# Attention's value products placed behind the next tile's scores and ahead of the transposes

## The reference

```python
scores = scale * np.matmul(q, k.transpose(0, 1, 3, 2)) + bias     # per head, 576 x 576
attn = np.exp(scores - max); attn = attn / (attn.sum(-1, keepdims=True) + 1e-9)
x = np.matmul(attn, v)                                            # B, S, H*D = 4, 576, 512
logits = x @ w_gate; gate = sigmoid(x @ w_local)
# per batch, token by token: the expert is argmax(logits), or the previous token's where gate >= 0.5
out[b, s] = p[e] * (relu(x[b, s] @ w1[e]) @ w2[e])
```

## Time and profile before

| what | value |
|---|---|
| median of 3 runs | 714.79 us (714.54 to 715.71) |
| the profiled execution | 715.85 us, of which the span of instructions is 714.1 us |
| PE busy | 658.3 us (92% of the span) |
| DVE, ACT, POOL busy | 376.8, 343.8, 194.1 us |
| copy_a on DVE (L813) | 686 ns each |
| copy_shared on ACT (L630) | 266 ns each |

### The profile page before, as it was taken

One profiled execution on the slowest core, in us unless ns is written; L12 is line 12 of the kernel. 1 busy time (PEld: TensorE's weight loads), 2 busy tenths in 40 slices (PEclk: granted clock), 3 DMA queues, 4 the chain that ended last, 5 costly groups with the idle time before them and its releaser, 6 DMA issues. The chain is left out here.

```text
span 714.1 us, 14144 instructions
## 1 busy us (share of the span) xinstructions
PE 658.3 (92%) x4353; PEld 528.3 (74%) x4353; DVE 376.8 (53%) x803; ACT 343.8 (48%) x727; POOL 194.1 (27%) x178
## 2 busy tenths in 40 slices
PE   6777899999999999999955899999999999999994
PEld 3224788888888888888735788888888888888883
DVE  5999565555555555556657642478424422122220
ACT  4997566666666666666530341466424422212221
POOL 4000614444444444445501011112111111111101
PEclk9999999999999999999975899999999999999998
DMA  7778534447444444444074941148310011111100
GB/s 166 202 195 206 109 68 100 99 97 212 98 100 96 99 97 98 98 101 94 18 264 151 344 152 64 45 154 308 104 44 31 35 44 44 44 44 44 44 0 1
DMA packets 67960, 77.05 MB, mean 108 GB/s; under 512 B 46543, under 2 KB 47055, under 8 KB 67920
## 3 DMA queue, kind: packets, MB, share of 16 engines
q1 hardware_dynamic: 63392, 64.58, 34.4%
q0 software_dynamic: 4144, 11.54, 5.1%
q10 hardware_dynamic: 384, 0.44, 0.2%
HBM read 69.06 MB, written 11.27 MB: 112 GB/s over the span
## 5 line engine op out<-in xcount | busy, mean ns | idle before, releaser
L790 DVE CUSTOM_DVE_ANT_0 sm<-ps_s,bias 128x576 f32<-128x576 f32 x128 | 91.7, 754 | 66.9 <-PE ps_s L1075 66.8
L610 ACT ACTIVATE sm<-sm,negmax 128x576 f32<-128x576 f32 x144 | 111.9, 778 | 5.7 <-DVE negmax L790 5.6
L1250 PE MATMUL ps_pv<-w2hi,hThi 128*128 128x512 f32 x200 | 80.5, 402 | 1.4 <-DVEq L979 1.4
L999 DVE TENSOR_TENSOR hTlo<-ps_s,hThi 128x512 fp32r<-128x512 f32 x50 | 32.2, 686 | 92.8 <-ACT hThi L724 92.6
L1250 PE MATMUL ps_pv<-w2hi,hTlo 128*128 128x512 f32 x200 | 78.3, 391 | 0.0
L1250 PE MATMUL ps_pv<-w2lo,hThi 128*128 128x512 f32 x200 | 77.9, 390 | 0.0
L1146 PE MATMUL ps_pv<-pT,vt 128*64 128x320 f32 (+1 forms) x512 | 69.1, 410 | 4.5 <-issue 0.7
L506 POOL CAST ksplit<-raw 128x1152 fp32r<-128x1152 f32 x15 | 17.2, 1147 | 195.8 <-DMA raw<-in_kq_dram 195.7
L1227 PE MATMUL ps_s<-w1hi,xThi 128*128 128x512 f32 x200 | 64.9, 406 | 4.9 <-DVE xTlo L971 3.1
L716 ACT ACTIVATE hsb<-ps_s 128x512 f32<-128x512 f32 x25 | 15.0, 599 | 110.6 <-PE ps_s L1227 104.6
L558 POOL DMA_INDIRECT out_dram<-ysb,sidx x25 | 25.5, 1020 | 156.5 <-ACT ysb L731 156.5
(11 more groups left out here) (184 smaller groups left out, 1293.0 us busy)
## 6 DMA issues: line engine op xcount, KB each, us to landing
w1raw<-in_moe_w_dram SPq DMA_DIRECT2D x18, 1024.0 KB
w2raw<-in_moe_w_dram SPq DMA_DIRECT2D x18, 1024.0 KB
raw<-in_kq_dram SPq DMA_DIRECT2D x32, 432.0 KB, 5.1
bias<-stage SPq DMA_DIRECT2D x32, 288.0 KB, 3.2
raw<-in_kq_dram SPq DMA_DIRECT2D x32, 128.0 KB, 4.9
vt<-in_v_dram SPq DMA_DIRECT2D x32, 128.0 KB, 2.4
tokens_dram<-xl SPq DMA_DIRECT2D x64, 64.0 KB, 1.7
bias_tail<-stage SPq DMA_DIRECT2D x4, 144.0 KB, 2.4
```

Source lines behind the costliest of these rows:

```text
L610: nc.scalar.activation(probs, probs, ACT.Exp, scale=-1.0, bias=negmax[:, u % 2, hd:hd + 1], accum_out=sums[:, pr % 2, 2 * t + hd:2 * t + h ...
L790: nc.vector.tensor_tensor_reduce(sm[:, u % 2, S * hd:S * (hd + 1)].rearrange("p (a c) -> p a c", a=2), ps_s[:, hd, :, 0:HALF], bias.rearra ...
L999: V.tensor_tensor(hTlo[:, 4 * i:4 * i + 4, :].rearrange("p k t -> p (k t)"), ps_s[:, 1, i, :], hThi[:, 4 * i:4 * i + 4, :].bitcast(F32).re ...
L1250: last = nc.tensor.matmul(ps_pv[:], h[:, f, :], w[:, f, :], start=f == 0 and h is hThi and w is w2hi, stop=f == KF - 1 and h is hTlo)
```

## The change

On PE the two value groups move by one iteration: group 1 of the pair before goes from the end of iteration t = 0 to t = 1, and group 0 from t = 2 to t = 3, and in both cases to a place between scores(u + 1) and the turns of u. turn_probs is cut in three functions. At t = 1 and 3 their order becomes first, second, shared; elsewhere it stays first, shared, second. Each of the functions turn_second and turn_shared now has its own wait on the second exponential (exped), and in turn_shared that wait stands ahead of the one on copied_s. On ACT, iterations t = 1 and 3 take the exponentials of u + 1 first, then the value copies, copy_b(u) and copy_shared(u). DVE, POOL and SP keep their streams.

```diff
--- before.py
+++ after.py
@@ -650,18 +650,27 @@
                 nc.scalar.copy((pv1[:], pv2[:, P:3 * P])[g], ps_pv[:, TAIL:TAIL + 2 * P]).then_inc(pv_copied, 1)
             for u in range(-1, ITEMS + 2):
                 pr, t = tile_of_item(u)
-                if t == 1 and pr:
-                    copy_values(pr - 1, 1)
-                if t == 3 and 0 <= pr < NPAIR:
-                    copy_values(pr, 0)
-                if 0 <= u < ITEMS:
-                    copy_shared(u)
-                if u + 1 < ITEMS:
-                    exponential(u + 1, 0)
-                if 0 <= u < ITEMS and t < FULL:
-                    copy_b(u)
-                if u + 1 < ITEMS and (u + 1) % QT < FULL:
-                    exponential(u + 1, 1)
+                if t in (1, 3):
+                    if u + 1 < ITEMS:
+                        exponential(u + 1, 0)
+                        if t + 1 < FULL:
+                            exponential(u + 1, 1)
+                    if t == 1 and pr:
+                        copy_values(pr - 1, 1)
+                    if t == 3:
+                        copy_values(pr, 0)
+                    if u < ITEMS:
+                        copy_b(u)
+                        copy_shared(u)
+                else:
+                    if 0 <= u < ITEMS:
+                        copy_shared(u)
+                    if u + 1 < ITEMS:
+                        exponential(u + 1, 0)
+                    if 0 <= u < ITEMS and t < FULL:
+                        copy_b(u)
+                    if u + 1 < ITEMS:
+                        exponential(u + 1, 1)
 
 
             act.wait_ge(route, 4)
@@ -1090,8 +1099,7 @@
                                                         stop=hd == 1 and part is qlo and o + n == HALF)
                     last.then_inc(scored, 1)
 
-            def turn_probs(u):
-                pr, t = tile_of_item(u)
+            def turn_first(u):
                 pe.wait_ge(exped, heads_done(u, 0))
                 if u:
                     pe.wait_ge(copied_a, u)
@@ -1099,13 +1107,26 @@
                     last = nc.tensor.transpose(ps_t[:, 0, P * kb:P * (kb + 1)], sm[:, u % 2, P * kb:P * (kb + 1)],
                                                ident[:])
                 last.then_inc(turned_a, 1)
+
+            def turn_second(u):
+                pe.wait_ge(exped, heads_done(u, 1))
+                if full_before(u):
+                    pe.wait_ge(copied_b, full_before(u))
+                for kb in range(FULL):
+                    last = nc.tensor.transpose(ps_t[:, 1, P * kb:P * (kb + 1)],
+                                               sm[:, u % 2, S + TAIL + P * kb:S + TAIL + P * (kb + 1)],
+                                               ident[:])
+                last.then_inc(turned_b, 1)
+
+            def turn_shared(u):
+                pr, t = tile_of_item(u)
+                pe.wait_ge(exped, heads_done(u, 1))
                 if u:
                     pe.wait_ge(copied_s, u)
                 if t in (1, 3) and u > 1:
                     pe.wait_ge(pv_copied, 2 * pr + t // 2)
                 o0 = 2 * P + 2 * TAIL
                 if t < FULL:
-                    pe.wait_ge(exped, heads_done(u, 1))
                     nc.tensor.transpose(ps_pv[:, o0:BANK], sm[:, u % 2, P * FULL:P * FULL + 2 * TAIL],
                                         ident[:]).then_inc(turned_s, 1)
                 else:
@@ -1114,14 +1135,6 @@
                         last = nc.tensor.matmul(ps_pv[:, o0 + D * hd:o0 + D * (hd + 1)], sm[:, u % 2, k0:k0 + P],
                                                 ident[:, D * hd:D * (hd + 1)], start=True, stop=True)
                     last.then_inc(turned_s, 1)
-                if t < FULL:
-                    if full_before(u):
-                        pe.wait_ge(copied_b, full_before(u))
-                    for kb in range(FULL):
-                        last = nc.tensor.transpose(ps_t[:, 1, P * kb:P * (kb + 1)],
-                                                   sm[:, u % 2, S + TAIL + P * kb:S + TAIL + P * (kb + 1)],
-                                                   ident[:])
-                    last.then_inc(turned_b, 1)
 
             def values(pr, g, done):
 
@@ -1163,15 +1176,22 @@
                 pr, t = tile_of_item(u)
                 if u + 1 < ITEMS:
                     scores(u + 1)
+                if t == 1 and pr:
+                    values(pr - 1, 1, 2 * pr - 1)
+                if t == 3 and 0 <= pr < NPAIR:
+                    values(pr, 0, 2 * pr)
                 if 0 <= u < ITEMS:
-                    turn_probs(u)
-                if t == 0 and pr:
-                    values(pr - 1, 1, 2 * pr - 1)
-                if t == 2 and 0 <= pr < NPAIR:
-                    values(pr, 0, 2 * pr)
+                    turn_first(u)
+                    if t in (1, 3):
+                        turn_second(u)
+                        turn_shared(u)
+                    else:
+                        turn_shared(u)
+                        if t < FULL:
+                            turn_second(u)
                 if t == 1 and pr:
                     turn_output(pr - 1, 1)
-                if t == 3 and 0 <= pr < NPAIR:
+                if t == FULL and 0 <= pr < NPAIR:
                     turn_output(pr, 0)
             pe.wait_ge(logged, NPAIR)
             pe.wait_ge(copied_a, ITEMS)
```

## The result

The changed kernel takes 704.55 us (702.18 to 706.21, 4 runs) where the kernel before took 714.66: that is 10.1 us faster by the medians, and the ratio of the two groups of runs is 0.9855 (0.9835 to 0.9874), which makes 10.4. From here on a time is followed by its ratio to the kernel before, measured beside it, with the 95% interval. The prediction said 711.5 us with a range from 707.5; the time lies outside it, on the fast side. A second group of runs of the same kernel gave 704.08 us and 0.9854 (0.9829 to 0.9880).

A forecast was written before the change was run, and what follows sets the result against it. The prediction took PE's own stream to set the pace (matmuls busy 269.2 of 288.0 us), so only its gaps could be gained. Terms: 4.9 - 0.7 - 1.5 - 0 + 0.6 = 3.3 us, median 714.79 to 711.5 us, range 707.5 to 715.6.

The forecast's parts named there:

- What stays: Stall at t = 0 after a pair's start: order said to be the same, so the stall was taken to stay.
- Entries of the value groups: Gap ahead of value products: 0.16 of 0.29 us gained 30 times, 0.05 in pair 0; 4.9 us in all.
- rival 1: Going from 128 to 64 columns needs no array drain; entry gain 8.7 us, time 707.7 us; chance 0.10.
- The sign that idle times from issue stay at the value products: At the value products' weight loads (L1146), idle times from issue stay in the changed profile, holding the drain.
- Exits: Value group now followed by the first turn instead of scores; shape changes as often as before, so 0.
- DVE in the scores of t = 2: Scores' second half waits for DVE's bias addition of t = 1: 0.10 us, 15 times, 1.5 us lost.
- The shared turn behind ACT's copies: Shared turn of t = 1 waits for ACT's value copies: 0.05 us, 15 times, 0.7 us lost; group 0 none.
- Waits and their order: Added or reordered waits at the second and shared turns: taken as 0, ends -1.6 and +1.6 us.
- Rival 2: Four or five waits ahead of a value group hold PE themselves; about 714.6 us; chance 0.20.
- First and last pair: Stalls in pair 0's shared turn of t = 2 and the last item's first turn go: 0.6 us gained together.
- POOL's slack, 2.8 us,: From the end of POOL's splits to the scores needing them: 2.8 us, against 0.2 taken from each period.
- My own signs: Wrong if the period doesn't fall, falls by more than 0.35, or anything outside attention moves by over 1 us.

The follow-up runs named there:

- e4: Kernel before with only ACT's order changed: at t = 4 the next pair's first exponential goes ahead of copy_shared; 707.77 us, 0.9903.
- e1: Changed kernel with the output block of group 0 put back in t = 3, behind the turns of t = 3; 713.46 us, 0.9974.
- e12: e5 without DVE's addition of 1e-9 to the denominators, the reciprocals reading the sums directly; 697.87 us, 0.9761.
- e6: Changed kernel with DVE's denominators and scale_x of group 0 one iteration later; 702.75 us, 0.9810.
- e3: Kernel before with the value groups alone moved on PE, order of turns, ACT and output block as before; 719.98 us, 1.0059.
- e9: Changed kernel on PE, with ACT's order of the kernel before; 713.07 us, 0.9976.
- e10: Changed kernel with the value groups alone back in their old places, all else as changed; 756.34 us, 1.0576.
- e8: Changed kernel with the output block back in t = 3 and ACT's first exponential ahead of copy_shared in t = 4; 713.78 us, 0.9975.
- e11: As e8, and DVE's denominators and scale_x of group 0 one iteration later; 698.05 us, 0.9766.
- e5: Changed kernel with SP's load of keys and queries issued one iteration earlier; 744.88 us, 1.0400.
- e0: Changed kernel run again unchanged, as the measure of its group of runs; 704.08 us.

## Why the prediction was wrong

The step that failed is "What stays": "The stall at t = 0 after a pair's start ... comes from the last item's shared copy, the first exponential behind it and the short item t = 4: that order is the same." The cause was named rightly (e4 shows it), but the order is not the same: the output block of group 0 moved into it. Its worth is 0.50 us a pair (e1 against the changed kernel), 6.5 us over 13 periods, and by the estimate above about 2.3 in the last, where it covers part of the slow addition too. The medians of e1 and the changed kernel are 8.9 us apart. It was priced at nothing since it was not read.

*Entries of the value groups: 0.16 forecast, 0.29 measured.* The mechanism was right, the size was not. The load stands 0.07 ahead of the scores' shown end, as taken:

```profile
253.53 0.52 PE L1096 MATMUL ps_s<-ksplit,qlo 128*128 128x288 f32 x3
...
253.98 1.49 PEld L1159 LDWEIGHTS ps_pv<-pT,vt 128*64 128x64 f32 x16
```

253.53 + 0.52 is 254.05, and all 31 groups behind scores have the same 0.07; that the change of shape costs this much in the third direction too was only assumed in the prediction. What was too small is the gap before: scores follow a second turn 0.36 us after its start (244.36 to 244.72 above), so the 0.72 us of the earlier trace rows, from the second turn at 242.63 to the first value product 0.03 behind its load, held a gap of 0.36, and I had 0.29, from a shared turn that follows a first one. After the scores the cost is 0.07. So 0.36 - 0.07, 30 times, is 8.7 us and not 4.9. It is chance that this is the number of rival 1, no drain: its sign, products that start 0.1 us or more before the scores' end, did not appear. The sign that idle times from issue stay at the value products, as the change of shape is in them, came true in part: 15 of 0.16 us stay, at group 1, which the profile names after copy_a here and issue in e12.

*Exits: forecast 0.* The first turn behind group 1 takes 0.05 us longer than behind scores, 0.06 a pair with what follows it (turns t = 1 in the table).

*DVE in the scores of t = 2: right.* Forecast 0.10 us, 15 times. Measured 0.12 (1.35 in the changed kernel, 1.23 in e6).

*The shared turn behind ACT's copies: no stall.* It starts 0.44 behind the second turn in the changed kernel, its own pace. The copies' lead was real though narrow: e3, with one turn less of cover, waits, and e9 and e10 show what it costs when ACT comes late.

*Waits and their order: forecast 0, ends 1.6.* In e1 the shared turn of t = 0 starts 0.76 us behind the first turn, 0.85 before: 0.09 us, of which the second turn loses 0.03 again. That is 1.0 to 1.4 us in 16 times, near the end of the range, on the good side. That the new order of the waits does it was not tested by itself. Rival 2 fell: a value group's four or five waits hide behind the scores, as the 0.07 in 31 of 31 shows.

*First and last pair: forecast 0.6.* The stalls went as said, 0.5 us in pair 0 (the shared turn of t = 2 starts 0.59 us behind the first turn instead of 1.11) and 0.3 at the last item. But at the start of pair 1 PE waits for POOL's split in either kernel, 2.0 us before and 2.5 in the changed one, so pair 0's part is given back there.

*POOL's slack, 2.8 us,* shrank more than by the period. From the end of a pair's split to its first scores there were 2.3 to 3.0 us in pairs 3 to 15; in the changed kernel's first profile there are 0.05 to 2.1, six of thirteen under 0.6, and at one pair PE waits (0.7 us). Why it shrank so much was not tried.

Without the output block the forecast's own kernel is e1: its period of 17.57 is 0.47 shorter where I said 0.2, its time 713.46. Inside my range, but by misses that cancel: a gain mis-sized, and losses at the last full period (3.5 us) and at POOL's split behind pair 0 not seen at all. That hit would have been luck.

My own signs said the same: "I am wrong ... if it falls by more than 0.35" of the period, and it fell by 0.97.

## What to carry to other kernels

Read every line of a diff for what it moves, a changed constant too: the smallest hunk here was worth 0.50 us a pair, the rest of the change, with the move in the title, 0.47. Where PE waits at a place where two queues are late by the same time, one engine's repair shows nothing (e8) until the other's is made (e11), or until work that is ready anyway is put there. And after a transfer is moved, look at what the engine behind it now runs beside: a gain of slack on POOL cost 40 us through one short DVE instruction (e5).

## What the runs showed of the hardware

- A DVE TENSOR_SCALAR on 128 x 9 numbers that takes 0.16 us took 2.05 to 2.41 us when it started behind a POOL TENSOR_TENSOR of 2.65 us (pairs 1 to 13 of e5), and ended 0.02 to 0.04 us behind it. With less of POOL's instruction left it took less (1.66 in the kernel before, 0.79 beside a CAST in the changed one). RECIPROCAL of 128 x 8 (0.19 us, 16 of 16 in e12) was not held.
- After a wait of PE of 1.9 to 2.0 us the granted clock of e5 fell to 1.2 GHz for about 3 us, nine times of nine. The length of the wait does not settle it: after 1.65 us in e1 it fell, after 1.6 us in e5 it fell once (pair 1) and stayed at full three times, and e10, which has waits of up to 1.6 us at the shared turn 27 times, keeps it at full from 90 to 400 us, as does e11 after a single wait of 2.0 us at 83 us. Two stretches of e5, each behind a wait of 1.6 us:

```profile
113.60:116.80 3.20, 3.20 (x14) 1.46 (x12) 0.85 (x4) 1.87 (x6) 0.00 (x0) 0.50 0.00 0
276.80:281.00 4.20, 4.20 (x28) 2.45 (x28) 2.56 (x7) 3.58 (x9) 0.00 (x0) 1.00 0.17 29
```

- The runs' scatter of 3 to 4 us has a source behind attention, as far as two profiles can tell. From the last value group to the end it is 355.1 us in the changed kernel's first profile and 357.6 in e0's. (Within attention e0's is 1.7 us the shorter, at the start of pair 1 and at the one wait for POOL's split, where it was expected.) Routing runs at 1.2 GHz. The clock rises at 382.1 us in the one profile and at 382.7 in the other, which is 36.7 and 39.0 us behind the last value group, and in e0's it falls once more, from 389.5 to 392.9. Two stretches at equal distances from the last value group, first of the one, then of the other:

```profile
374.40:385.40 11.00, 7.40 (x26) 5.80 (x27) 6.43 (x12) 0.59 (x1) 0.95 (x1) 0.65 0.52 176
385.40:395.40 10.00, 7.97 (x41) 6.27 (x40) 7.21 (x8) 5.83 (x8) 0.95 (x1) 1.00 1.04 391
```

```profile
372.70:383.70 11.00, 7.35 (x21) 5.58 (x20) 6.23 (x12) 0.58 (x1) 0.94 (x1) 0.55 0.49 181
383.70:393.70 10.00, 7.97 (x33) 6.17 (x32) 7.21 (x8) 5.83 (x8) 0.94 (x1) 0.83 0.93 341
```

The first profile of the changed kernel is its fastest run (702.18), the one of before 1.2 us over its median; so the two profiled executions are 13.7 us apart and the medians 10.1. What decides when the clock rises, and whether it falls again, was not tried.
